# The way back of an attention mix: identity and gate weights in one matmul, or a transpose and a matmul of 16 columns

## The chip, the cores and the metric

One Trainium2 chip, one core of it. The metric is the time of one launch in device microseconds (us). The kernel before took 448.68 us, the median of three runs (448.59 to 450.16).

## What is computed

Attention over a window of 128 keys, then a mixture of experts on its rows. Cut to what matters:

```python
# q, k, v: [4, 8, 576, 64]
scores = scale * q @ k.T + bias            # masked outside a window of 128
attn = softmax(scores)
x = (attn @ v).transpose(0, 2, 1, 3).reshape(2304, 512)
logits = x @ w_gate                        # [2304, 8]
expert = argmax(logits); gate = softmax(logits)[expert]
out[i] = gate[i] * (relu(x[i] @ w1[expert]) @ w2[expert])
```

Everything is float32. The choice of expert hangs on `logits`, so neither `x` nor the gate product may lose precision.

## The kernel before, in words

The kernel has two stages. In the attention stage (some 12 to 172 us of the profile) each of the 4 batches is cut into 5 units of queries, four of 128 rows and one of 64, and each unit into two quads of 4 heads: `STEPS` = 10 steps in a batch, 40 in all, numbered `kk` in a batch. The expert stage follows; its matmuls all stand on L1286, and the change touches nothing in it.

Every engine's order is written out by hand in a loop over the steps. In step `kk` TensorE (PE) does, in this order (`batch`, L1197):

1. `turn_q` or `turn_k` (L1104): four transposes of rows of a unit that is due two units later, into bank 7 of PSUM. It waits for `back_kept`, since bank 7 also holds the result of the way back.
2. `turn_probs` (L1139): eight transposes (four for the first unit) of the probabilities of this step.
3. `turn_back` (L1169) of the step before, the place of the change. It waits for `mixT_ready`, and ahead of it PE waits for the copy of what it turned in 1: `kT_ready` (VectorE, L769) in the odd steps, `qT_ready` (ScalarE, L609) in the even ones.
4. `score` (L1126) of two steps later: four matmuls.
5. `mix` (L1158): eight matmuls (four for the first unit) that give the mix of heads transposed, `mixT`, features on the partitions and queries in the columns.

`turn_back` brings the mix back to rows and forms the gate's partial products at once. The right operand `eye_wg` has 144 columns for each chunk of 128 features: the identity in 128 of them, and 16 columns of gate weights (2 heads x 8 experts, the rows of the other head being zero).

```python
back_ps = ps[:, 7, 0:2 * PAIR].rearrange("p (c n) -> p c n", c=2)   # PAIR = P + 2 * E = 144
for c in range(2):
    last = te.matmul(back_ps[0:rows[i], c, :], mixT[:, c, 0:rows[i]], eye_wg[:, 2 * quad + c, :], ...)
```

VectorE (DVE) then multiplies both parts with the inverse sums of the softmax (`normalise`, L789 and L795), which is also what frees bank 7 (`back_kept`). In each step DVE does: the copy of turned keys (L769, odd steps), its half of the copies of probabilities (L325), in odd steps `sums_eps` and `inv_sums` (L775, L777), `normalise`, and the four passes that add the bias and take the minimum (L757). ScalarE (ACT) copies `mixT` (L616), turned queries (L609), the other half of the probabilities (L621), and does the exponentials (L602).

GpSimd (POOL) builds the constants at the start, `eye_wg` among them (L474, L475), and later splits the first expert's weights in two parts, eight times a CAST (L506) and a TENSOR_TENSOR (L507), beside the attention. ACT waits for `eye_ready` before it issues the loads of the gate weights into `eye_wg` (L652); PE waits for these (`wg_landed`) once, in step 1.

How a float32 matmul shows in the profile: each one is two MATMUL rows with a weight load (LDWEIGHTS, engine PEld) each; a transpose is one of each. Call such a pair of load and MATMUL a pass. So `turn_back` is four passes in each step, 160 in all.

Of the kernel before, what the change touches and what calls it, by code (L numbers as in the profile page):

```python
# [24 lines left out]
ALU = mybir.AluOpType  # L25
# [3 lines left out]
P = 128  # L29
# [5 lines left out]
def attention_moe(nc, q, k, v, w_gate, w1, w2, capacity, out):  # L35
    B, H, S, DH = q.shape
    D, E = w_gate.shape
# [6 lines left out]
    DC, FC = D // P, F // P  # L44
# [4 lines left out]
    PAIR = P + 2 * E  # L49
# [10 lines left out]
    rows = [min(P, S - P * i) for i in range(TI)]  # L60
# [9 lines left out]
    with ctx:  # L70
        def sb(name, shape, dt=F32):
            return ctx.enter_context(nc.sbuf_tensor(name, shape, dt))
# [9 lines left out]
        def sem(name):  # L82
            return ctx.enter_context(nc.semaphore(name))
# [25 lines left out]
        inv_sums = sb("inv_sums", [P, TI, H])  # L109
        eye_wg = sb("eye_wg", [P, DC, PAIR])  # L110
        gate_part = sb("gate_part", [P, H, E])
# [136 lines left out]
        early_kept = sem("early_kept")  # L248
        eye_ready = sem("eye_ready")
        x_ready = sem("x_ready")  # L250
# [201 lines left out]
        def _(pool):  # L452
            steps = [0]

            def link(ins):

                steps[0] += 1
                ins.then_inc(pool_step, 1)
                pool.wait_ge(pool_step, steps[0])
# [13 lines left out]

            link(g.memset(eye_wg[:, :, :], 0.0))  # L474
            g.affine_select(out=eye_wg[:, :, 0:P], in_=eye_wg[:, :, 0:P], compare_op=ALU.not_equal, fill=1.0,  # L475
                            base=0, pattern=[[0, DC], [-1, P]], channel_multiplier=1).then_inc(eye_ready, 1)

# [115 lines left out]
        def _(act):  # L593
# [55 lines left out]
            nc.scalar.activation(mins[:, 0, 0:1], ident[:, 0:1], ACT.Exp)  # L649
            act.wait_ge(eye_ready, 1)  # L650
            for part in range(2):
                act.dma_start(eye_wg[DH * part:DH * part + DH, :, P + E * part:P + E * part + E],  # L652
                              w_gate.rearrange("(c t p) e -> t p c e", t=2, p=DH)[part]).then_inc(wg_landed, 16)
# [437 lines left out]
        def _(pe):  # L1091
# [72 lines left out]
            def turn_back(b, kk):  # L1164

                i, quad = divmod(kk, 2)
                pe.wait_ge(mixT_ready, b * STEPS + kk + 1)
                for c in range(2):
                    last = te.matmul(back_ps[0:rows[i], c, :], mixT[:, c, 0:rows[i]], eye_wg[:, 2 * quad + c, :],  # L1169
                                     start=True, stop=True)  # L1170
                last.then_inc(turned_back, 1)
# [237 lines left out]
```

## Time and profile before

| | |
|---|---|
| median of 3 runs | 448.68 us |
| profiled execution, its own time | 449.06 us |
| span of the profile | 447.4 us |
| PE busy | 422.8 us, 95% |
| DVE, ACT, POOL busy | 279.3, 217.6, 98.6 us |
| share of PE in the chain that ended last | 86% |
| all passes of L1169 | 29.0 us busy, 160 of them |

The span leaves out what lies around the program's instructions: the profiled execution took 1.7 us more than its span. Matmuls are pipelined, so that the durations of neighbours overlap: what a pass costs in a stream is the distance from one start to the next, not its duration.

### The profile page before, as it was taken

How to read it: one execution, taken by the hardware profiler on the slowest of the kernel's cores; microseconds unless marked ns; L12 is line 12 of the kernel's file. 1: busy time of each engine (PE TensorE's matmuls, PEld its weight loads, DVE VectorE, ACT ScalarE, POOL GpSimd, SP SyncE). 2: the span in 40 equal slices, each digit the busy share in tenths (PEclk: the TensorE clock that was granted, in tenths of full speed). 3: DMA queues.
4: the chain of work that ended last, by engine and by line, in shares of the span. 5: the costliest groups of instructions: out<-in, count | busy, mean ns of one | idle time of the engine just before them, and what ended most of it. 6: DMA issues, size and time to landing. Idle time of an engine off the chain costs nothing.

```text
span 447.4 us, 11059 instructions
## 1 busy us (share of the span) xinstructions
PE 422.8 (95%) x2860; PEld 342.1 (76%) x2861; DVE 279.3 (62%) x829; ACT 217.6 (49%) x576; POOL 98.6 (22%) x154
## 2 busy tenths in 40 slices
PE   6999999999999989799999999999999999999982
PEld 6777687777777767688888888888888888888871
DVE  4887778778879776676776634662667766432230
ACT  3777677676677671434455515422444555111100
POOL 5092065000501201222122222222111122222201
PEclk9999999999999999999999999999999999999997
DMA  9997299269631111166566651660656664111100
GB/s 175 242 257 190 70 270 225 73 195 228 147 74 46 49 26 37 48 235 219 177 206 213 201 180 50 225 234 26 216 188 193 216 206 134 47 47 37 36 35 15
DMA packets 78861, 63.59 MB, mean 142 GB/s; under 512 B 61614, under 2 KB 61614, under 8 KB 78832
## 3 DMA queue, kind: packets, MB, share of 16 engines
q1 hardware_dynamic: 71504, 51.66, 41.1%
q0 software_dynamic: 3520, 10.76, 7.5%
q10 hardware_dynamic: 3808, 0.80, 1.1%
q8 instruction: 15, 0.25, 0.2%
q14 instruction: 14, 0.11, 0.1%
HBM read 53.77 MB, written 10.23 MB: 143 GB/s over the span
## 4 chain that ended last, share of the span: by engine, by line
PE 86%; DVE 7%; DMA 2%; ACT 1%; issue 1%; SPq 0%; POOL 0%; DVEq 0%; POOLq 0%
PE ps L1286 52%; PE ps L1126 7%; PE ps L1158 7%; PE ps L1169 5%; PE ps L1139 4%; PE ps L1303 4%; PE ps L1104 3%; DVE probs L757 2%; PE ps L1279 2%; DMA q_rows<-in_q 2%; DVE kT L769 1%; ACT qT L609 1%; DVE sums_eps L775 1%; PE ps L1193 1%; DVE probsT L325 0%
## 5 line engine op out<-in xcount | busy, mean ns | idle before, releaser
L1286 PE MATMUL ps<-weights_sb,rowsT_hi 128*128 (+1 forms) x336 | 107.8, 402 | 1.4 <-DVE rowsT_lo L1024 1.4
L1286 PE MATMUL ps<-weights_sb,hiddenT_hi 128*128 x320 | 98.6, 389 | 1.2 <-DVE hiddenT_lo L1017 1.2
L695 ACT ACTIVATE hidden<-ps 128x512 f32<-128x512 f32 x20 | 11.9, 597 | 139.7 <-PE ps L1286 100.7
L1037 DVE TENSOR_TENSOR weights_sb<-raw,weights_sb 128x1024 f32 (+1 forms) x56 | 67.2, 1221 | 15.7 <-issue 10.9
L602 ACT ACTIVATE probs<-probs,mins 128x256 f32<-128x256 f32 (+2 forms) x160 | 73.7, 467 | 0.0
L1286 PEld LDWEIGHTS ps<-weights_sb,rowsT_hi 128*128 128x128 f32 x336 | 61.1, 188 | 15.2 <-DVE rowsT_lo L1024 1.6
L1286 PEld LDWEIGHTS ps<-weights_sb,hiddenT_hi 128*128 128x128 f32 x320 | 60.0, 188 | 14.0 <-issue 1.4
L1286 PE MATMUL ps<-weights_sb,rowsT_lo 128*128 (+1 forms) x168 | 66.2, 394 | 0.0
L1286 PE MATMUL ps<-weights_sb,hiddenT_lo 128*128 x160 | 62.4, 390 | 0.0
L1017 DVE TENSOR_TENSOR hiddenT_lo<-ps,hiddenT_hi 128x512 fp32r<-128x512 f32 x40 | 25.8, 686 | 58.0 <-ACT hiddenT_hi L699 58.0
L684 ACT ACTIVATE weights_sb<-raw 128x1024 f32 (+1 forms) x56 | 56.6, 1067 | 0.0
L757 DVE CUSTOM_DVE_ANT_0 probs<-ps,bias 128x256 f32<-128x256 f32 (+2 forms) x160 | 51.7, 378 | 6.2 <-PE ps L1126 5.8
L552 POOL DMA_INDIRECT out<-y_sb,dst_now x20 | 20.3, 1015 | 154.3 <-DVE y_sb L1044 154.3
L1126 PE MATMUL ps<-kT,qT 64*128 64x256 f32 (+2 forms) x320 | 39.9, 368 | 1.0 <-DVE kT L769 1.0
L1158 PE MATMUL ps<-probsT,v_rows 128*64 128x128 f32 (+2 forms) x576 | 40.5, 272 | 0.1
L1158 PEld LDWEIGHTS ps<-probsT,v_rows 128*64 128x64 f32 (+1 forms) x576 | 30.1, 135 | 13.1 <-issue 9.6
L1286 PEld LDWEIGHTS ps<-weights_sb,rowsT_lo 128*128 128x128 f32 x168 | 31.5, 187 | 7.7
L1169 PE MATMUL ps<-eye_wg,mixT 128*128 128x144 f32 (+1 forms) x160 | 29.0, 304 | 7.8 <-DVE kT L769 4.8
L1139 PE MATMUL ps<-ident,probs 128*128 128x128 f32 (+2 forms) x288 | 35.7, 264 | 0.0
L1286 PEld LDWEIGHTS ps<-weights_sb,hiddenT_lo 128*128 128x128 f32 x160 | 30.0, 188 | 6.3
L1044 DVE TENSOR_SCALAR y_sb<-ps,weight_now 128x512 f32<-128x512 f32 x20 | 15.0, 751 | 30.2 <-PE ps L1286 29.9
L325 DVE COPY probsT<-ps 128x512 f32<-128x512 f32 (+3 forms) x48 | 23.8, 509 | 15.4 <-PE ps L1139 15.3
(152 smaller groups left out, 532.5 us busy)
## 6 DMA issues: line engine op xcount, KB each, us to landing
raw<-in_moe_w SPq DMA_DIRECT2D x64, 512.0 KB, 3.8
q_rows<-in_q SPq DMA_DIRECT2D x16, 256.0 KB, 5.7
v_rows<-in_v SPq DMA_DIRECT2D x16, 256.0 KB, 4.3
x_rows<-x_sb SPq DMA_DIRECT2D x16, 256.0 KB, 4.1
k_rows<-in_k SPq DMA_DIRECT2D x13, 256.0 KB, 5.7
k_rows<-in_k ACTq DMA_DIRECT2D x3, 256.0 KB, 5.8
q_rows<-in_q SPq DMA_DIRECT2D x4, 128.0 KB, 4.1
k_rows<-in_k SPq DMA_DIRECT2D x4, 128.0 KB, 4.4
```

The lines of the kernel that those rows point to most:

```text
L325: last = copy(dst[0:size, lo:hi, :, 0:rows[i]], src[0:size, lo:hi, :, 0:rows[i]])
L552: g.indirect_dma_start(out, bass.IndirectOffsetOnAxis(ap=dst_now[j][:, 0:1], axis=0), y_sb[j][:, :], None, bounds_check=N - 1, oob_is_err= ...
L602: last = nc.scalar.activation(pr, pr, ACT.Exp, bias=mins[0:rows[i], kk % 2, n:n + 1], scale=-1.0, accum_out=sums[0:rows[i], i, h:h + 1])
L684: nc.scalar.activation(weights_sb[:, bass.ds(e & 1, 1), 2 * layer, RAW * j:RAW * (j + 1)] .rearrange("p s n -> p (s n)"), raw[:, j, :], AC ...
L757: last = vec.tensor_tensor_reduce(out=probs[0:rows[i], kk % 2, n, 0:keys[i]], in0=src, in1=bias[0:rows[i], head(quad, n), shift:shift + ke ...
L1017: vec.tensor_tensor(hiddenT[1][:, 4 * half:4 * half + 4, :], hiddenT_ps(half).rearrange("p (c s) -> p c s", c=4), upper, ALU.subtract).the ...
L1037: vec.tensor_tensor(weights_sb[:, slot, 2 * layer + 1, part].rearrange("p s n -> p (s n)"), raw[:, j, :], weights_sb[:, slot, 2 * layer, p ...
L1126: ins = te.matmul(scores_ps(kk % 2, odd)[0:rows[i], 256 * n:256 * n + keys[i]], qT[part, i, h // 2, 0:rows[i]], kT[part, h // 2, first_key ...
L1139: last = te.transpose(probsT_ps(odd)[0:size, at:at + rows[i]], probs[0:rows[i], kk % 2, 2 * odd + n, P * blk:P * blk + size], ident[0:rows ...
L1158: last = te.matmul(mixT_ps[DH * odd:DH * odd + DH, n, 0:rows[i]], v_rows[0:size, tile, DH * h:DH * h + DH], probsT[0:size, blk, 2 * odd + ...
L1169: last = te.matmul(back_ps[0:rows[i], c, :], mixT[:, c, 0:rows[i]], eye_wg[:, 2 * quad + c, :], start=True, stop=True)
L1286: ins = te.matmul(dst, left[a], right[c], start=first and n == 0, stop=last and n == 2)
```

## The change

`turn_back` now first turns the two chunks of `mixT` back with two transposes against `ident`, the identity that the other transposes use, and then multiplies each chunk with the 16 columns of gate weights alone, in matmuls of their own, into the columns behind. The results lie where they lay. The table `eye_wg` is replaced by `wg_pairs`, which has the 16 columns for each of four chunks; POOL only clears it, and the building of four identities is gone. The rest of the diff renames the semaphore.

```diff
-        eye_wg = sb("eye_wg", [P, DC, PAIR])
+        wg_pairs = sb("wg_pairs", [P, DC, 2 * E])
...
-            link(g.memset(eye_wg[:, :, :], 0.0))
-            g.affine_select(out=eye_wg[:, :, 0:P], in_=eye_wg[:, :, 0:P], compare_op=ALU.not_equal, fill=1.0,
-                            base=0, pattern=[[0, DC], [-1, P]], channel_multiplier=1).then_inc(eye_ready, 1)
+            g.memset(wg_pairs[:, :, :], 0.0).then_inc(wg_cleared, 1)
...
-            act.wait_ge(eye_ready, 1)
+            act.wait_ge(wg_cleared, 1)
             for part in range(2):
-                act.dma_start(eye_wg[DH * part:DH * part + DH, :, P + E * part:P + E * part + E],
+                act.dma_start(wg_pairs[DH * part:DH * part + DH, :, E * part:E * part + E],
                               w_gate.rearrange("(c t p) e -> t p c e", t=2, p=DH)[part]).then_inc(wg_landed, 16)
...
                 pe.wait_ge(mixT_ready, b * STEPS + kk + 1)
+                back = back_ps
                 for c in range(2):
-                    last = te.matmul(back_ps[0:rows[i], c, :], mixT[:, c, 0:rows[i]], eye_wg[:, 2 * quad + c, :],
+                    te.transpose(back[0:rows[i], c, 0:P], mixT[:, c, 0:rows[i]], ident[:, :])
+                for c in range(2):
+                    last = te.matmul(back[0:rows[i], c, P:PAIR], mixT[:, c, 0:rows[i]], wg_pairs[:, 2 * quad + c, :],
                                      start=True, stop=True)
                 last.then_inc(turned_back, 1)
```

On PE the order of a step in the second unit of a batch reads, before:

```order
L1104 MATMUL ps<-ident,k_rows 128x64 x4
L1139 MATMUL ps<-ident,probs 128x128 x8
L1169 MATMUL ps<-eye_wg,mixT 128x144 x2
L1126 MATMUL ps<-kT,qT 128x256 x4
L1158 MATMUL ps<-probsT,v_rows 64x128 x8
```

and now:

```order
L1102 MATMUL ps<-ident,k_rows 128x64 x4
L1137 MATMUL ps<-ident,probs 128x128 x8
L1168 MATMUL ps<-ident,mixT 128x128 x2
L1170 MATMUL ps<-wg_pairs,mixT 128x16 x2
L1124 MATMUL ps<-kT,qT 128x256 x4
L1156 MATMUL ps<-probsT,v_rows 64x128 x8
```

Two rows stand where one stood; nothing changed its place, and the same holds in all 40 steps. In passes, four became six: two of a transpose, four of a matmul.

On POOL the start reads, before:

```order
L471 AFFINE_SELECT maskadd<-maskadd 128x256
L474 MEMSET eye_wg 128x576
L475 AFFINE_SELECT eye_wg<-eye_wg 128x4x128
L479 IOTA iota_e 128x8
```

and now:

```order
L471 AFFINE_SELECT maskadd<-maskadd 128x256
L474 MEMSET wg_pairs 128x64
L477 IOTA iota_e 128x8
```

One instruction is gone and one is smaller; ACT's loads of the gate weights wait for the last of these.

## Rows read from the trace of the kernel before

**Rows 1.** The page: busy time of the engines, and PE's clock in 40 slices.

```profile
PE 422.8 (95%) x2860; PEld 342.1 (76%) x2861; DVE 279.3 (62%) x829; ACT 217.6 (49%) x576; POOL 98.6 (22%) x154
...
PEclk9999999999999999999999999999999999999997
```

**Rows 2.** The chain that ended last, 12 to 172 us, its shares by line.

```profile
by line: PE ps L1126 20.6%; PE ps L1158 18.3%; PE ps L1169 15.3%; PE ps L1139 12.1%; PE ps L1104 9.3%; DVE probs L757 6.6%; DVE kT L769 3.8%; issue 2.4%; ACT qT L609 2.3%; DVE sums_eps L775 1.9%; DVE probsT L325 1.3%; DVE x_sb L789 0.8%; PE
```

**Rows 3.** Timeline of PE, two steps: start us, us, engine, line, what, count.

```profile
62.73 0.76 PE L1169 MATMUL ps<-eye_wg,mixT 128*128 128x144 f32 x4
63.42 1.13 PE L1126 MATMUL ps<-kT,qT 64*128 64x256 f32 x8
...
66.83 0.66 PE L1169 MATMUL ps<-eye_wg,mixT 128*128 128x144 f32 x4
67.42 1.13 PE L1126 MATMUL ps<-kT,qT 64*128 64x256 f32 x8
```

**Rows 4.** The chain in order of time, pieces of PE: start us, us, what.

```profile
148.45 0.22 PE ps L1139 x2
148.67 0.49 PE ps L1169 x4
...
149.19 0.34 PE ps L1177 x14
```

**Rows 5.** Timeline of weight loads: the first two of four blocks (L1169, L1104, L1169).

```profile
22.77 0.30 PEld L1169 LDWEIGHTS ps<-eye_wg,mixT 128*128 128x128 f32 x2
...
21.33 0.20 PEld L1104 LDWEIGHTS ps<-ident,k_rows 128*128 128x128 f32 x2 [0.17 <-issue]
...
47.23 0.19 PEld L1169 LDWEIGHTS ps<-eye_wg,mixT 128*64 128x64 f32 x2 [0.33 <-DVE kT L769]
```

**Rows 6.** A group of weight loads by shape: busy us, mean ns | idle before.

```profile
L1169 PEld LDWEIGHTS ps<-eye_wg,mixT 128*128 128x128 f32 x128 | 17.4, 189 | 10.3 <-DVE kT L769 6.0 <-DVE rowsT_lo L880 1.6 <-issue 0.8
```

**Rows 7.** Timeline of weight loads: four transposes of 64 rows of queries.

```profile
65.51 0.33 PEld L1104 LDWEIGHTS ps<-ident,q_rows 64*128 64x128 f32 x4 [0.17 <-issue]
```

**Rows 8.** Timeline of PE: a way back of the unit of 64 rows.

```profile
50.91 0.70 PE L1169 MATMUL ps<-eye_wg,mixT 128*64 128x144 f32 x4 [0.25 <-ACT qT L609]
51.54 0.70 PE L1126 MATMUL ps<-kT,qT 64*128 64x256 f32 x4
```

**Rows 9.** Timeline of DVE, POOL and PE about 31 to 34 us.

```profile
31.01 2.37 POOL L507 TENSOR_TENSOR weights_sb<-raw,weights_sb 128x1024 fp32r<-128x1024 f32 x1
...
31.67 1.73 DVE L775 TENSOR_SCALAR sums_eps<-sums 128x8 f32<-128x8 f32 x1
...
34.26 0.33 PE L1104 MATMUL ps<-ident,q_rows 128*128 128x128 f32 x1 [0.65 <-DVE gate_part L795]
```

**Rows 10.** The same about 71 to 74 us, and POOL and DVE about 63 us.

```profile
71.63 1.46 DVE L775 TENSOR_SCALAR sums_eps<-sums 128x8 f32<-128x8 f32 x1
...
73.94 0.33 PE L1104 MATMUL ps<-ident,q_rows 128*128 128x128 f32 x1 [0.38 <-DVE gate_part L795]
...
62.71 1.04 POOL L506 CAST weights_sb<-raw 128x1024 fp32r<-128x1024 f32 x1
63.83 2.37 POOL L507 TENSOR_TENSOR weights_sb<-raw,weights_sb 128x1024 fp32r<-128x1024 f32 x1
...
63.47 0.31 DVE L775 TENSOR_SCALAR sums_eps<-sums 128x8 f32<-128x8 f32 x1
```

**Rows 11.** Timeline of ACT at the start.

```profile
4.44 0.20 ACT L649 ACTIVATE mins<-ident 128x1 f32<-128x1 f32 x1
4.57 1.37 ACTq L652 DMA_DIRECT2D eye_wg<-in_moe_w_gate  x2
```

**Rows 12.** Timeline of PE at the start.

```profile
1.63 3.54 PE L1258 MATMUL ps<-ident 128*128 128x128 f32 x16 [1.63 <-POOL ident L463]
5.54 0.66 PE L1104 MATMUL ps<-ident,q_rows 128*128 128x128 f32 x4 [0.37 <-DMA q_rows<-in_q]
6.03 0.60 PE L1104 MATMUL ps<-ident,k_rows 128*128 128x128 f32 x4
```

More of the change, by code:

```diff
@@ L248, in attention_moe @@
         early_kept = sem("early_kept")
-        eye_ready = sem("eye_ready")
+        wg_cleared = sem("wg_cleared")
         x_ready = sem("x_ready")
```

## The prediction

> **What bounds the kernel now.** I read the page first, then the chain of waits for the attention stage, then the timeline of single steps, and last the groups of weight loads. On the page the reader is to see that TensorE (PE) is busy for 95% of the span and that its granted clock stays at the upper of its two levels, 2.4 GHz, up to the last slice [rows 1]. The chain shows the same for the stage that the change touches: of the 160 us from 12 to 172, PE's five lines hold 75.6%, and the way back alone, L1169, 15.3% [rows 2]. Of its 40 blocks I count 37 in the chain. So what a block gets longer or shorter, the stage mostly does too. It is not enough to compare durations, since passes overlap. The prices below are distances between starts.
>
> **What one block costs now.** A block that follows on without a wait takes 0.49 us for four passes, 0.122 each, while a transpose takes 0.11 [rows 4]. From its first start to that of the next block, at L1126, are 0.59 us, as from 66.83 to 67.42 [rows 3]; so 0.10 goes to handing over to `score`, whose operands have another shape. A block that begins after a wait takes 0.69, as from 62.73 to 63.42 [rows 3]: its first weight load isn't hidden. How long a load occupies the array can be read there. The second load starts when the first matmul starts, when the first load is done. Two loads of 0.19 span 0.30, so the second began 0.11 after the first; for a transpose the same reading gives 0.20 less 0.14, 0.06; for the unit of 64 rows 0.19 less 0.136, 0.054 [rows 5]. This is what the diff doesn't show: **the load of a float32 matmul takes 0.108 for 128 columns of weights, twice that of a transpose, and it takes this whatever the matmul moves**. Now it hides behind the 144 columns moved: the loads last 189 ns by their mean, and yet a pass takes 0.122 [rows 4, 6].
>
> **What a block costs after the change.** Two transposes, 0.22. Then four passes with 16 columns, each still with a load of its own. Moving 16 columns takes 16/144 of 0.122, 0.014, too short to hide a load of 0.108: the pass is as long as its load. How much above the load a pass lies that its load bounds is seen in transposes that move 64 columns: (0.33 - 0.14)/3 = 0.063 for a load of 0.057 [rows 5, 7]. So I take 0.108 + 0.006 = 0.114. After a wait: first load 0.057, transpose 0.109, transpose with the first gate load behind it 0.114, three more passes 0.342, the last stream 0.014, handing over 0.09: 0.73 for 0.69, **+0.04**. Without a wait the first load is hidden in both, and it is 0.67 for 0.59, **+0.09**. In the unit of 64 rows (two steps of ten) it is 0.63 now [rows 8]; loads are half as long, a gate pass takes about 0.062, and the sum is 0.03 + 0.109 + 0.109 + 0.186 + 0.014 + 0.09 = 0.54, **-0.10**.
>
> No row shows a float32 pass of 16 columns, so both ends are kept. Below: a pass of 0.063, as if the gate loads were as quick as those of transposes [rows 7]; further off, 0.024, as in the bf16 matmuls of 8 to 48 columns [rows 4]. Above: 0.122, as now, whatever is moved or loaded [rows 4]. I take 0.114, since the 0.108 under it is measured on the very operand that is loaded, `mixT`.
>
> **The sum.** Of the 37 blocks in the chain, 24 are of full rows and begin after a wait, 5 without one (pieces of 0.49 like that in rows 4), 8 are of 64 rows. Not all of it arrives. About 31.7 us DVE's `sums_eps` lies for 1.73 us instead of 0.16 and ends when POOL's TENSOR_TENSOR ends; PE then waits 0.65 for bank 7 [rows 9]. POOL's work there starts when the raw weights land, not when PE is ready. What the four blocks ahead add (3 x 0.04 + 0.09 = 0.21) only makes this stall shorter. The same stands at 71.6 us, with 0.38 of waiting [rows 10]. POOL's second group is set off by a load that waits for the end of the first batch, so only the three blocks since then count, 0.17, and they vanish too. Left are 19 x 0.04 + 3 x 0.09 - 8 x 0.10 = 0.76 + 0.27 - 0.80 = **+0.2 us**. The three blocks off the chain stand beside DVE work (the two stalls, and the choice of the expert's top at 98 us) and cost nothing; without that cover they would add 0.2.
>
> The other edits. POOL's second constant falls away and ACT may issue the gate loads sooner, but ACT is busy with its first ACTIVATE until 4.64 and issues from 4.57 [rows 11]: nothing to gain, and the cover is that instruction. DVE reads the result as before, 0.04 to 0.09 later, in a step where it sits idle for longer than that. 40 x 2 more passes have to be issued; a pass of 0.024 [rows 4] shows that issuing isn't a limit. No queue of transfers and no other wait moves.
>
> Against the profiled execution of 449.06 the sum gives 449.3; that execution lies 0.4 above the median shown. Against the median it is 448.68 + 0.22 = **448.9 us**.
>
> **The rivals.**
> *A, gate passes as cheap as they look.* What speaks for it: 16 columns for 144. If a gate pass costs 0.063, a full block is 0.12 (0.08) shorter than now: 19 x 0.12 + 3 x 0.08 + 0.8 = 3.4 us gained, 445.3; with 0.024 some 443. Against it stand the loads of 0.108 [rows 5]. The Trainium skill, page "Perfetto Trace Analysis", section "Transposes", asks that a logical transpose be a transpose and not a standard matmul; by it the change is an improvement, and 445.3 is its time. It leaves out that the operand must now be loaded twice. I give A 8%.
> *B, a fixed price for each pass.* If a pass costs 0.122 whatever it loads, a block after a wait gets 0.07 longer, one without 0.12, and the unit of 64 rows gains nothing and gets 0.09 longer: 19 x 0.07 + 3 x 0.12 + 8 x 0.09 = 2.4, **451.1 us**. It decides from the point where a pass of 16 columns and 64 columns of weights costs more than 0.12. For it: every pass of L1169 takes 0.122 now, with 64 columns of weights too. Against it: 144 columns moved explain that, and the transposes show 0.063 [rows 7]. I give B 12%.
> *C, the clock falls.* After the change PE moves 0.43 us less by matmul in a step and more by transpose. If transposes don't keep the clock up, PE falls from 2.4 to 1.2 GHz. A transpose at the lower level takes 3.54/16 = 0.22, as the sixteen of the start show [rows 12]; twice the PE share of rows 2 would be 120 us more, 569. But those sixteen are all that PE had done, and right behind them four transposes take 0.49 with their first load, 0.11 each: transposes alone raised the clock [rows 12]. The Trainium skill, page "TensorE: Matmul & The Clock Gate", section "Part 4: PE-mode transpose", says that the upper level isn't reached by transposes, which don't count as busy; by that rule the time is that of C, and the trace disagrees. 2%.
> *D, another meeting with POOL.* At 63.47 `sums_eps` waits 0.15 for the end of a CAST; the next TENSOR_TENSOR starts at 63.83 [rows 10]. If DVE came 0.3 later it would lie behind all 2.37 of it. I expect 0.04 later. The stall of 1.57 at 31.7 cost PE 0.65, so this one would cost about 1.4, 450.3: within the bound of no difference. It is part of the forecast's 78% and widens its range.
>
> **How the numbers follow.** The forecast's own terms give 448.4 (a pass of 0.109: 19 x 0.02 + 3 x 0.06 - 0.8 = -0.3) to 449.6 (0.122 for full rows only: +0.9), and D adds up to 1.4; the three runs shown reach from 448.6 to 450.2, so chance alone can move the time by half a microsecond. I take 447.5 to 451.0 for 8 in 10; it leaves out A, C and most of B. What differs by 0.5%, 2.2 us, can be told from no change: faster than 446.4 is A, 8%; slower than 450.9 is B and C, 14%; the rest, 78%, is no difference.
>
> **What would show it.** The gate passes' loads should have a mean of about 189 ns (136 for 64 rows) and begin 0.11 apart, the whole block with the two transposes taking 0.67 or 0.73, and 0.54 in the unit of 64 rows. Passes 0.06 apart are A, 0.122 in the unit of 64 rows too is B. PE's clock should stay up. The stall near 31.7 should be 0.2 shorter and end at the same time. The shares of DVE and ACT should not move. I would be wrong most if the load of a narrow matmul is not the 0.108 that I read off a first load, or if the blocks of 64 rows gain nothing.

## The result, and the profile after

The changed kernel takes 452.89 us, the median of 18 runs (449.54 to 455.13); the kernel before took 449.1 us beside it (18 runs, 448.04 to 450.16). The ratio is 1.0073, with a 95% interval of 1.0051 to 1.0095. The quotient of the medians is 1.0084, that of the means 1.0074. So it is slower by 0.73%, more than the bound of no difference (0.5%), and the time lies above the predicted range.

| | before | after |
|---|---|---|
| median | 449.1 us | 452.89 us |
| profiled execution, its own time | 449.06 us | 455.13 us |
| span of the profile | 447.4 us | 453.4 us |
| PE busy | 422.8 us | 429.3 us |
| mean granted clock of PE in it | 0.994 | 0.985 |

The page of the kernel after:

```profile
span 453.4 us, 11217 instructions
...
PE 429.3 (95%) x2940; PEld 350.9 (77%) x2941; DVE 279.5 (62%) x829; ACT 217.6 (48%) x576; POOL 99.4 (22%) x153
...
PEclk9999999999999986999999999999999999999998
```

The shares of the engines stand where they stood [rows 1], and so do the shares of the chain from 12 to 172 us; the way back, now two lines, has 15.5% of it (15.3% in [rows 2]):

```profile
by line: PE ps L1124 20.6%; PE ps L1156 18.1%; PE ps L1137 12.7%; PE ps L1102 9.3%; PE ps L1168 7.8%; PE ps L1170 7.7%; DVE probs L755 6.6%; DVE kT L767 3.8%; issue 2.3%; ACT qT L607 2.3%; DVE sums_eps L773 1.9%; DVE probsT L325 1.4%; DVE x
```

What is new is an 8 and a 6 in the line of the clock, in slices 15 and 16 of 40, some 160 to 180 us: there TensorE ran at the lower of its two levels for part of the time. The kernel before shows nothing like it.

So there are two effects, and the timeline of the two profiled executions keeps them apart. I compare the start of the same way back in both:

| step (of 40, from 0) | before | after | difference |
|---|---|---|---|
| 34 | 154.03 | 155.54 | +1.5 |
| 35 | 159.72 | 161.26 | +1.5 |
| 36 | 163.16 | 166.24 | +3.1 |
| 38 | 168.67 | 171.94 | +3.3 |
| first matmul behind the stage | 174.20 | 180.34 | +6.1 |
| end of the span | 447.4 | 453.4 | +6.0 |

At the first way back of all, ahead of any new block, the difference is 0.16 (15.06 for 14.90). So up to 160 us the longer blocks have made at most 1.35. Then come two jumps, of 1.5 and of 2.9, and behind the stage the difference stays the same. Both jumps are stretches at the lower level. Windows of the kernel after (stretch, length; busy us and count of PE, PEld, DVE, ACT, POOL; then granted clock, transfers' share and GB/s):

```profile
157.00:163.00 6.00, 4.62 (x50) 3.54 (x48) 3.85 (x16) 3.42 (x11) 1.21 (x2) 1.00 0.00 0
163.10:166.40 3.30, 3.30 (x24) 2.97 (x20) 1.21 (x9) 1.15 (x3) 0.00 (x0) 0.50 0.32 80
166.50:173.20 6.70, 6.70 (x83) 5.28 (x81) 5.38 (x25) 4.62 (x22) 0.00 (x0) 1.00 0.12 43
173.40:180.00 6.60, 6.60 (x25) 4.82 (x24) 2.13 (x11) 0.28 (x1) 0.00 (x0) 0.50 0.09 20
```

and of the kernel before, at the same places of the program:

```profile
155.50:161.50 6.00, 4.62 (x50) 3.46 (x48) 3.93 (x16) 3.42 (x11) 1.19 (x2) 1.00 0.01 3
161.50:164.90 3.40, 3.40 (x42) 2.76 (x40) 2.70 (x15) 2.36 (x9) 0.00 (x0) 1.00 0.30 78
164.90:171.40 6.50, 6.47 (x74) 4.73 (x70) 4.33 (x23) 3.79 (x17) 0.00 (x0) 1.00 0.11 42
```

The eighth number is to be read. It is 0.50, 1.2 GHz, for 3.4 us from 163.0, and for 6.8 us from 173.3. Beside the first numbers it is instructive: ahead of the first fall PE was busy for 4.62 of 6.00 us in both kernels, and ahead of the second one for 6.70 of 6.70. **By the busy share nothing was amiss; the clock fell all the same, and only after the change.** What a fall costs is read in the timeline around the first. After:

```profile
161.26 0.44 PE L1168 MATMUL ps<-ident,mixT 128*128 128x128 f32 x2 [1.38 <-DVE rowsT_lo L878]
161.53 0.52 PE L1170 MATMUL ps<-wg_pairs,mixT 128*128 128x16 f32 x4
...
162.78 1.77 PE L1156 MATMUL ps<-probsT,v_rows 128*64 128x128 f32 x16
164.48 1.97 PE L1137 MATMUL ps<-ident,probs 128*128 128x128 f32 x8
166.24 0.49 PE L1168 MATMUL ps<-ident,mixT 128*128 128x128 f32 x2
```

The same place before:

```profile
161.20 1.09 PE L1158 MATMUL ps<-probsT,v_rows 128*64 128x128 f32 x16
162.23 1.09 PE L1139 MATMUL ps<-ident,probs 128*128 128x128 f32 x8
163.16 0.66 PE L1169 MATMUL ps<-eye_wg,mixT 128*128 128x144 f32 x4
```

From start to start the mix takes 1.70 us and the eight transposes 1.76, for 1.03 and 0.93 before. That is 1.5 more, all of the first jump.

The block itself, in the kernel after, first of full rows, then of 64 rows:

```profile
23.00 0.44 PE L1168 MATMUL ps<-ident,mixT 128*128 128x128 f32 x2
23.27 0.52 PE L1170 MATMUL ps<-wg_pairs,mixT 128*128 128x16 f32 x4
23.72 0.49 PE L1124 MATMUL ps<-kT,qT 64*128 64x256 f32 x2
...
51.45 0.41 PE L1168 MATMUL ps<-ident,mixT 128*64 128x128 f32 x2 [0.25 <-ACT qT L607]
51.78 0.40 PE L1170 MATMUL ps<-wg_pairs,mixT 128*64 128x16 f32 x4
52.12 0.49 PE L1124 MATMUL ps<-kT,qT 64*128 64x256 f32 x2
```

From start to start the first takes 0.72, 0.69 before [rows 3], and the second 0.67, 0.63 before [rows 8]. The block of 64 rows got longer, where I had forecast 0.10 less. Its weight loads say why:

```profile
22.99 0.20 PEld L1168 LDWEIGHTS ps<-ident,mixT 128*128 128x128 f32 x2
23.16 0.53 PEld L1170 LDWEIGHTS ps<-wg_pairs,mixT 128*128 128x128 f32 x4
...
51.44 0.14 PEld L1168 LDWEIGHTS ps<-ident,mixT 128*64 128x64 f32 x2 [0.49 <-ACT qT L607]
51.78 0.31 PEld L1170 LDWEIGHTS ps<-wg_pairs,mixT 128*64 128x64 f32 x4 [0.20 <-issue]
```

With full rows the first gate load begins at 23.16, while the second transpose is still moving. With 64 rows the transposes' loads end at 51.58 and the next begins only at 51.78, with 0.20 us in which nothing is loaded. By an estimate from 0.11 for a transpose, the second one begins to move at 51.56 and is through at 51.67, 0.11 ahead of that load.

The passes themselves cost what was forecast. Their loads, in groups by shape (busy us, mean ns | idle before), stand beside the 189 of [rows 6]:

```profile
L1170 PEld LDWEIGHTS ps<-wg_pairs,mixT 128*128 128x128 f32 x128 | 16.8, 192 | 0.0
...
L1170 PEld LDWEIGHTS ps<-wg_pairs,mixT 128*64 128x64 f32 x32 | 2.7, 146 | 1.8 <-issue 1.8
```

How far apart they begin is read from the block above: four of them (0.53) less the last one's 0.19 make three distances of 0.113; with 64 rows (0.31 - 0.146)/3 makes 0.055. The 1.8 us of idle time in the second group, over the 8 blocks of 64 rows, are the gap: 0.2 each.

Of the 18 runs 8 had a mean granted clock of 0.993 or more; they took 449.54 to 451.75, a median of 450.1, 1.0 above the kernel before (two of them, at 451.7, stand apart, and no trace of them was kept). Five had 0.987 or 0.988 and took 452.86 to 454.13. Five had 0.984 or 0.985 and took 454.29 to 455.13. **The longer passes cost about 1.0 us, and the 10 runs of 18 with a lower clock took 2.8 to 5.0 more (3.0 and 4.6 by the medians of the two groups).** The median, 452.89, is that of a time with three values; the experiments had to say where both costs come from.

### The profile page after: what moved, and what is told of

Read it like the earlier page. It is cut to its first block, busy times and chain, and to the rows that moved or that the text cites. A ratio compares the mean times of both kernels' runs of the same rounds, so it can differ in the third digit from the quotient of the medians.

```text
span 453.4 us, 11217 instructions
## 1 busy us (share of the span) xinstructions
PE 429.3 (95%) x2940; PEld 350.9 (77%) x2941; DVE 279.5 (62%) x829; ACT 217.6 (48%) x576; POOL 99.4 (22%) x153
## 2 busy tenths in 40 slices
DMA packets 78862, 63.61 MB, mean 140 GB/s; under 512 B 61614, under 2 KB 61614, under 8 KB 78832
## 4 chain that ended last, share of the span: by engine, by line
PE 87%; DVE 7%; DMA 2%; ACT 1%; issue 1%; SPq 0%; POOL 0%; DVEq 0%; POOLq 0%
PE ps L1287 52%; PE ps L1124 7%; PE ps L1156 7%; PE ps L1137 5%; PE ps L1304 4%; PE ps L1102 3%; PE ps L1168 3%; PE ps L1170 3%; DVE probs L755 2%; PE ps L1280 2%; DMA q_rows<-in_q 2%; DVE kT L767 1%; ACT qT L607 1%; DVE sums_eps L773 1%; PE ps L1194 1%
## 5 line engine op out<-in xcount | busy, mean ns | idle before, releaser
L1287 PE MATMUL ps<-weights_sb,rowsT_hi 128*128 (+1 forms) x336 | 109.6, 408 | 1.4 <-DVE rowsT_lo L1022 1.4
L1035 DVE TENSOR_TENSOR weights_sb<-raw,weights_sb 128x1024 f32 (+1 forms) x56 | 67.2, 1220 | 15.5 <-issue 8.8
L1287 PEld LDWEIGHTS ps<-weights_sb,rowsT_hi 128*128 128x128 f32 x336 | 62.1, 191 | 15.3 <-DVE rowsT_lo L1022 1.6
L1156 PE MATMUL ps<-probsT,v_rows 128*64 128x128 f32 (+2 forms) x576 | 41.5, 276 | 0.1
L1137 PE MATMUL ps<-ident,probs 128*128 128x128 f32 (+2 forms) x288 | 36.7, 268 | 0.0
L1137 PEld LDWEIGHTS ps<-ident,probs 128*128 128x128 f32 (+2 forms) x288 | 30.0, 139 | 2.2 <-issue 1.5
```

The source lines that it names most:

```text
L1035: vec.tensor_tensor(weights_sb[:, slot, 2 * layer + 1, part].rearrange("p s n -> p (s n)"), raw[:, j, :], weights_sb[:, slot, 2 * layer, p ...
L1137: last = te.transpose(probsT_ps(odd)[0:size, at:at + rows[i]], probs[0:rows[i], kk % 2, 2 * odd + n, P * blk:P * blk + size], ident[0:rows ...
L1156: last = te.matmul(mixT_ps[DH * odd:DH * odd + DH, n, 0:rows[i]], v_rows[0:size, tile, DH * h:DH * h + DH], probsT[0:size, blk, 2 * odd + ...
L1287: ins = te.matmul(dst, left[a], right[c], start=first and n == 0, stop=last and n == 2)
```

## The experiments

The theory behind the first four: the gate passes cost what their loads cost (1.0 us), and the clock falls where too little is moved through the array, near 163 and 173 us. Its rivals: the clock falls by chance wherever the kernel has become longer, or because of the longer stage ahead of it.

In tables "fell" counts the runs with a mean granted clock under 0.992. A fall of 3.4 us to the lower level takes 3.4 x 0.5 / 450 = 0.004 from the mean, and runs without one lie at 0.993 to 0.996, so a run of 0.992 or 0.993 can hide one short fall; only the profiled runs show it for certain. Each kernel's runs stand beside runs of the kernel before on the same chip.

**e1: the new form in the last batch alone.** Batches 0 to 2 have the old form. In this one and in the others with both forms the table stays `eye_wg`, and the gate weights are its last 16 columns.

```diff
+                if b == B - 1:
+                    for c in range(2):
+                        te.transpose(back_ps[0:rows[i], c, 0:P], mixT[:, c, 0:rows[i]], ident[:, :])
+                    for c in range(2):
+                        last = te.matmul(back_ps[0:rows[i], c, P:PAIR], mixT[:, c, 0:rows[i]],
+                                         eye_wg[:, 2 * quad + c, P:PAIR], start=True, stop=True)
+                else:
+                    for c in range(2):
+                        last = te.matmul(back_ps[0:rows[i], c, :], mixT[:, c, 0:rows[i]],
+                                         eye_wg[:, 2 * quad + c, :], start=True, stop=True)
```

> The old way back in batches 0 to 2, the new one in the last batch alone. The trace of the changed kernel has the granted clock at its lower level for 3.4 us from 163.0 and for 6.8 us from 173.3, both at the end of the last batch, which the trace of before has not. Theory 1 (the new way back keeps PE less occupied with moving, and at the end of the last batch, where PE waits for VectorE and there are no more scores, that lets the clock fall): runs scatter as those of the changed kernel do, from about 449 to 454 us, and a share of them has a mean granted clock of 0.988 or 0.985 instead of 0.994. Rival 2 (the falls need the whole of the changed kernel, since all of it runs later or is moved against the chip's own rhythm): hardly any falls, 449.0 to 449.7 us. Rival 3 (a disturbance of those runs that has nothing to do with the kernel): the runs of before beside these fall as often.

**e2: the new form in batches 0 to 2, the old one in the last.** The same edit with `b < B - 1`.

> The complement: the new way back in batches 0 to 2, the old one in the last batch. Theory 1: no falls, mean clock 0.994 in every run, and only the longer blocks stay: three quarters of the 1.4 us by which the changed kernel is behind at 154 us, so before plus 1.0 to 1.2, about 450.2 us, with a scatter like that of before. Rival 2: falls in a share of the runs, up to 454 us.

| | median (range) | runs | ratio | fell |
|---|---|---|---|---|
| e1, new in the last batch | 451.59 (449.52 to 452.71) | 6 | 1.0037 (1.0017 to 1.0058) | 4 |
| e2, old in the last batch | 450.25 (449.91 to 450.85) | 4 | 1.0015 (1.0003 to 1.0028) | 0 |

A quarter of the new blocks brings the falls (451.54 to 452.71 in the four runs that fell, 449.52 and 449.85 in the two that did not), and three quarters of them elsewhere bring none. The profile of e1, by windows:

```profile
160.00:169.80 9.80, 9.80 (x119) 7.85 (x119) 7.62 (x39) 6.07 (x26) 0.00 (x0) 1.00 0.19 55
170.00:176.60 6.60, 6.60 (x24) 4.75 (x22) 2.04 (x11) 0.28 (x1) 0.00 (x0) 0.50 0.10 22
```

PE was busy for all of 9.80 us ahead of this fall. So the new form in the last batch alone is enough for a fall, and longer blocks ahead of it aren't needed. That falls stand nowhere else is not shown: e2 has only four runs, and the profiles of e4, e9 and e10 below each have a fall in batch 2, from 114.1, 130.7 and 112.3. e2 shows the price of the passes alone: +0.6 for three quarters of the blocks.

Its profile says little about the stalls. `sums_eps` starts at 31.84 and lies for 1.47 instead of 1.73, and PE then waits 0.30 for bank 7 instead of 0.65. But e1, whose first three batches are the old ones, has 1.51 and 0.42 there: the stall moves by 0.2 from one execution to the next without any change. At 71.6 PE waits in neither. Instead `sums_eps` of e2 lies for 1.71 at 63.61, and PE waits 0.41: that is rival D.

**e3: the old form for the units of 64 rows.** `if rows[i] == P:` the new form, else the old one.

> The new way back for units of 128 rows, the old one for the units of 64 rows, in all batches. In the changed kernel a block of 64 rows takes 0.675 us against 0.634 before, where I had forecast 0.54: 8 blocks, so this should give back about 0.3 us. If the blocks of 64 rows are also what lets the clock fall the second time (two of them stand right before 173.3), the runs with a fall should get rarer or have only the shorter one, and the median should come down to 450 to 451 us. If it is the full ones as well, the median stays at 452 to 453.

**e4: the gate matmuls of all units in the full array.** In the units of 64 rows, 128 columns of `mixT` are loaded as weights, and 128 rows written.

```diff
-                    last = te.matmul(back[0:rows[i], c, P:PAIR], mixT[:, c, 0:rows[i]], wg_pairs[:, 2 * quad + c, :],
+                    last = te.matmul(back[:, c, P:PAIR], mixT[:, c, :], wg_pairs[:, 2 * quad + c, :],
```

> The changed kernel, but in the units of 64 rows the gate matmuls load all 128 columns of the mix and write all 128 rows (the lower 64 are never read). In the changed kernel's trace there is a gap of 0.09 us between the last transpose and the first gate load in these blocks, and none in the full ones. Theory (the gap is a change of the array's shape: a float32 matmul with 64 columns of weights is run in half the array, the transposes in all of it): the gap is gone, the gate passes are 0.111 apart instead of 0.058, and the block takes about 0.66 to 0.70 us. Rival (the transpose of 64 columns itself ends late): the gap stays, and the block takes about 0.79 us.

e3 took 450.87 (6 runs, 449.84 to 452.55), ratio 1.0035 (1.0018 to 1.0051); two fell. Two of 6 can't be told from 10 of 18, so that the share of the blocks of 64 rows in the falls stays open. Its blocks of 64 rows are back at 0.63. Its profiled execution, in which the clock did not fall, shows the meeting with POOL that I had called rival D. POOL, DVE and PE about 64 to 67 us:

```profile
63.92 2.36 POOL L507 TENSOR_TENSOR weights_sb<-raw,weights_sb 128x1024 fp32r<-128x1024 f32 x1
63.96 2.35 DVE L775 TENSOR_SCALAR sums_eps<-sums 128x8 f32<-128x8 f32 x1
...
67.16 0.46 PE L1104 MATMUL ps<-ident,q_rows 64*128 64x64 f32 x4 [1.05 <-DVE gate_part L795]
```

DVE's `sums_eps` began 0.04 us behind POOL's instruction and lay for all of it; PE waited 1.05.

e4 was run once: 454.87 us, with the clock down for 3.4 us from 114.1 and for 6.8 from 172.2. It met POOL as e3 did, `sums_eps` lying for 2.00 at 63.60 and PE waiting 0.70. Its block of 64 rows is what it was made for:

```profile
50.92 0.41 PE L1168 MATMUL ps<-ident,mixT 128*64 128x128 f32 x2 [0.25 <-ACT qT L607]
51.16 0.52 PE L1170 MATMUL ps<-wg_pairs,mixT 128*128 128x16 f32 x4
51.61 0.49 PE L1124 MATMUL ps<-kT,qT 64*128 64x256 f32 x2
```

The gap between the last transpose and the first gate load is gone: the gate passes begin 0.24 after the transposes, not 0.33. With twice the columns to load, the four passes then take 0.45 up to `score`, not 0.34, and so the block is 0.69 in all. The 0.09 belongs to the step from a transpose to a float32 matmul with 64 columns of weights, not to the transposes of 64 rows, which are the same in e4. The Trainium skill, page "TensorEngine Tiling (Array Packing)", section "Key Properties", says that changing the tiling mode drains TensorE, and its section "Restrictions" that column tiling rules out the transpose mode for FP32 input. The two together would put a gap just here, and the trace has one, of 0.09 us. No row names a mode of the array, so that the gap is shown and its reading as a drain is not.

**What lets the clock fall: three candidates.** 1a: transposes don't keep the clock up, and the new form replaced matmuls by transposes. 1b: what is moved through the array keeps it up, by transposes too, but loading weights does not; the gate passes load for 0.11 and, by the prediction's estimate, move for 0.014. 1c: being busy keeps it up, whatever PE does. Beside these stands the plain rival that only the length of the stage counts. e5 and e6 fill the four steps ahead of and between the falls with passes that move much, and e7 adds passes that only load.

**e5: sixteen transposes more**, four in each of the steps 5 to 8 of the last batch, into a part of bank 7 that nobody reads.

```diff
                 pe.wait_ge(mixT_ready, b * STEPS + kk + 1)
                 back = back_ps
+                if b == B - 1 and 5 <= kk <= 8:
+                    for _ in range(4):
+                        te.transpose(ps[:, 7, 3 * P:4 * P], ident[:, :], ident[:, :])
```

> The changed kernel, and in the last batch's ways back of steps 5 to 8 four transposes of the identity more each, into columns that nobody reads, after the waits and so on PE's path: 16 passes of 0.109, +1.7 us for any theory. Theory 1a (transposes do not keep the clock up): falls as often as in the changed kernel (10 of 18 runs) or more, median 454 to 456. Theory 1b (what a pass moves keeps it up, a transpose too, and the gate passes fail because they mostly load): falls get rare, most runs at 451.5 to 452.5 with a mean clock of 0.993 to 0.996.

**e6: eight matmuls of 128 columns more** in the same places, the same time by other passes.

```diff
+                    for _ in range(2):
+                        te.matmul(ps[:, 7, 3 * P:4 * P], ident[:, :], ident[:, :], start=True, stop=True)
```

> The same as the run with filling transposes, with two float32 matmuls of 128 columns (four passes, 0.109 each) in the place of each four transposes: the same time added, the same columns moved. Theories 1a and 1b both expect hardly any falls, 451.5 to 452.5 us; if falls stay as frequent here, neither holds and the clock doesn't hang on what PE moves at the end of the batch.

**e7: the gate matmuls twice** in all steps of the last batch.

```diff
-                for c in range(2):
+                for c in (0, 1, 0, 1) if b == B - 1 else (0, 1):
                     last = te.matmul(back[0:rows[i], c, P:PAIR], mixT[:, c, 0:rows[i]], wg_pairs[:, 2 * quad + c, :],
```

> The changed kernel, and in the last batch each gate matmul is done twice: 10 blocks of 4 passes more at 0.111 (0.058 for 64 rows), +4.0 us. PE is busier by the clock on the wall, but what is added is loading. Theory 1c (being busy keeps the clock up, whatever PE does): falls get rare, 454 to 455 us. Theories 1a and 1b (loading doesn't count): every run or nearly every run falls, and more of the stretch is slow: 458 us or more, mean clock 0.985 or lower.

| | median (range) | runs | ratio | fell |
|---|---|---|---|---|
| after | 452.89 (449.54 to 455.13) | 18 | 1.0073 (1.0051 to 1.0095) | 10 |
| e5, transposes added | 452.81 (451.73 to 453.48) | 6 | 1.0072 (1.0053 to 1.0092) | 0 |
| e6, matmuls added | 453.05 (451.91 to 453.86) | 6 | 1.0081 (1.0060 to 1.0101) | 0, one at 0.992 |
| e7, gate matmuls doubled | 458.08 (456.52 to 460.70) | 6 | 1.0199 (1.0168 to 1.0230) | 6 |

The two windows of 10 us about the second fall tell the same. Of e5:

```profile
163.00:173.00 10.00, 10.00 (x118) 8.48 (x117) 6.75 (x34) 6.20 (x26) 0.00 (x0) 1.00 0.17 50
173.20:183.30 10.10, 10.08 (x92) 7.34 (x90) 6.38 (x35) 1.00 (x3) 1.47 (x2) 1.00 0.09 15
```

and of e7:

```profile
163.00:173.00 10.00, 10.00 (x118) 8.54 (x116) 6.52 (x32) 6.20 (x27) 0.00 (x0) 1.00 0.13 34
173.20:183.30 10.10, 10.10 (x53) 7.19 (x53) 3.40 (x17) 0.45 (x3) 0.00 (x0) 0.50 0.10 27
```

The first lines can hardly be told apart: the same busy time, and the same number of matmuls and loads within one. In a full step the added passes take the same 0.44 us in both. What differs is what they move, 128 columns in the added passes of e5 and 16 in those of e7. Behind the one the clock stays, behind the other it falls, for 10.1 us, and so it went in all runs, 0 of 6 against 6 of 6. This is 1b. 1a is refuted by e5: by it the falls should have stayed as frequent as after the change. The matmuls of e6 did as well, but for one run of 0.992, which may hide a short fall. 1c is refuted by e7, where PE was as busy. The length of the stage isn't it either: it is longer in e5 than after the change, and no run of e5 fell.

e5 is longer than a run of the kernel after that kept its clock by more than its added passes. Those take 0.44 in each of four steps, 1.75; the profiled execution was already 1.1 us behind after's at 147 us, ahead of all of them. Of that, 0.57 was there at its first way back, at 15.63 us. It then met POOL, and PE waited 1.01 for bank 7 at 27 us, as e6's did with 0.67; that is the meeting of [rows 9] at another step, and later waits differ too. Neither is made by the added passes.

**e8: the kernel before without `sums_eps`.** Was the meeting with POOL worth something in the kernel before? The reciprocal is taken of the sums directly.

```diff
-                vec.tensor_scalar(sums_eps[0:r, i, :], sums[0:r, i, :], 1e-9, None, ALU.add).then_inc(sum_step, 1)
-                dve.wait_ge(sum_step, b * 2 * TI + 2 * i + 1)
-                vec.reciprocal(inv_sums[0:r, i, :], sums_eps[0:r, i, :]).then_inc(sum_step, 1)
+                vec.reciprocal(inv_sums[0:r, i, :], sums[0:r, i, :]).then_inc(sum_step, 1)
```

> The kernel before without the addition of 1e-9 to the sums of exponentials (a sum is at least 1, so that the addition changes no bit); the reciprocal reads the sums themselves. In the traces the addition lay behind POOL's weight splitting for 0.5 to 2.3 us, and cost PE up to 1.1 us in one place and 0.4 to 0.65 in others. Theory (it is this instruction that is held while POOL works): the stalls of 0.65 and 0.38 us in the trace of before are gone, and the short wait between the two operations too: 1.0 to 1.5 us less than before, 448.2 to 448.7, and less scatter. Rival (the reciprocal is held in its place): no change.

It took 448.12 us (12 runs, 447.62 to 448.79), ratio 0.9973 (0.9963 to 0.9984), and in six more runs later the same 448.12, ratio 0.9972 (0.9960 to 0.9984):

> The kernel without the addition of 1e-9 once more, on the same chip as the run with the new order, so that the two can be compared: 0.25 to 0.3% below before, 12 runs within 1.2 us of one another.

POOL and DVE in the profile of e8, at the place of [rows 9]:

```profile
31.17 2.37 POOL L507 TENSOR_TENSOR weights_sb<-raw,weights_sb 128x1024 fp32r<-128x1024 f32 x1
...
31.45 0.19 DVE L775 RECIPROCAL inv_sums<-sums 128x8 f32<-128x8 f32 x1
```

The reciprocal begins inside POOL's instruction and takes 0.19. It is not held, where the TENSOR_SCALAR was held for 1.73. Where the time was won is seen by setting the ways back of the two profiled executions beside each other. e8 is 0.22 ahead at the first one, ahead of any stall; 0.94 behind the wait of 0.65 at 34 us, 1.40 behind that of 0.38 at 74 us [rows 9, 10], and 1.41 at the end of the stage. So it is the two waits, 0.7 and 0.45; the small instruction that each unit does without on DVE wins nothing elsewhere.

**e9: the order transpose, gate, transpose, gate.** If a gate load can hide behind a transpose that moves, each of the two should have one.

```diff
                 for c in range(2):
                     te.transpose(back[0:rows[i], c, 0:P], mixT[:, c, 0:rows[i]], ident[:, :])
-                for c in range(2):
                     last = te.matmul(back[0:rows[i], c, P:PAIR], mixT[:, c, 0:rows[i]], wg_pairs[:, 2 * quad + c, :],
```

> The changed kernel with the four operations of the way back in another order: transpose of the first chunk, its gate matmul, transpose of the second, its gate matmul, instead of both transposes and then both matmuls. Theory (a gate pass is as long as its weight load of 0.108 unless a transpose's moving of 0.107 lies over that load): two loads are hidden now instead of one, at the price of one short load of a transpose that isn't: a block of 128 rows after a wait takes 0.67 instead of 0.72 us (0.688 with the old way back), one without a wait 0.61 instead of 0.665 (0.586). A block of 64 rows changes the array's shape three times instead of once and takes about 0.85 instead of 0.675. Rival (the order doesn't matter, every pass has its price): 0.72, 0.665 and 0.675 as in the changed kernel.

```profile
22.68 0.33 PE L1168 MATMUL ps<-ident,mixT 128*128 128x128 f32 x1
22.85 0.29 PE L1169 MATMUL ps<-wg_pairs,mixT 128*128 128x16 f32 x2
22.99 0.30 PE L1168 MATMUL ps<-ident,mixT 128*128 128x128 f32 x1
23.13 0.29 PE L1169 MATMUL ps<-wg_pairs,mixT 128*128 128x16 f32 x2
23.35 0.49 PE L1124 MATMUL ps<-kT,qT 64*128 64x256 f32 x2
...
47.43 0.30 PE L1168 MATMUL ps<-ident,mixT 128*64 128x128 f32 x1 [0.17 <-DVE kT L767]
47.66 0.29 PE L1169 MATMUL ps<-wg_pairs,mixT 128*64 128x16 f32 x2
47.88 0.30 PE L1168 MATMUL ps<-ident,mixT 128*64 128x128 f32 x1
48.11 0.29 PE L1169 MATMUL ps<-wg_pairs,mixT 128*64 128x16 f32 x2
48.33 0.38 PE L1124 MATMUL ps<-kT,qT 64*128 64x128 f32 x2
```

This is PE's timeline of e9, a single run of 458.68 us with a mean clock of 0.972 (down for 10.2 us from 130.7 and again from 175.1). A full block takes 0.67, 0.02 less than before the change [rows 3] and 0.05 less than after it. The block of 64 rows goes three times from a transpose to a narrow matmul or back and takes 0.90. The full block loads as much in less time, and in this run the clock fell for longer, which cost more than the order won; one run doesn't show that the order made it so.

**e10: e8 and this order for the full units of batches 0 to 2; e12: for batches 0 and 1 only.** The last batch, and all units of 64 rows, keep the old form.

```diff
                 for c in range(2):
+                    if b < B - 1 and rows[i] == P:
+                        te.transpose(back_ps[:, c, 0:P], mixT[:, c, :], ident[:, :])
+                        last = te.matmul(back_ps[:, c, P:PAIR], mixT[:, c, :], eye_wg[:, 2 * quad + c, P:PAIR],
+                                         start=True, stop=True)
+                    else:
+                        last = te.matmul(back_ps[0:rows[i], c, :], mixT[:, c, 0:rows[i]],
+                                         eye_wg[:, 2 * quad + c, :], start=True, stop=True)
```

> The kernel before without the addition of 1e-9, and with the way back as transpose, gate matmul, transpose, gate matmul, but only for units of 128 rows of batches 0 to 2; units of 64 rows and the whole last batch, where the clock is at stake, keep the one matmul of 144 columns. If a block after a wait takes 0.67 for 0.688 and one without 0.61 for 0.586: 18 x 0.02 - 3 x 0.03 = 0.25 us less than without the addition alone, 0.3% and a little below before; no falls of the clock. If the loads aren't hidden by the order: 0.7 us more than without the addition alone.

> The last kernel (no addition of 1e-9; transpose, gate matmul, transpose, gate matmul) with the new way back in batches 0 and 1 alone. One of its five runs had the clock down for 3.4 us from 112.3, right behind the step of batch 2 in which PE waits 1.1 us for VectorE's routing work, and took 449.75 us instead of 447.5 to 448.0. If the clock falls where a wait and the new way back come together, no run falls now, since in batches 0 and 1 there is no such wait: all runs within 447.5 to 448.3 us. If the falls come by chance with the new way back anywhere, one or two of the runs are at 449.5 or more.

| | median (range) | runs | ratio | fell |
|---|---|---|---|---|
| e8, no `sums_eps` | 448.12 (447.62 to 448.79) | 12 | 0.9973 (0.9963 to 0.9984) | 0 |
| e10, and in turn in batches 0 to 2 | 447.80 (447.49 to 449.75) | 5 | 0.9961 (0.9947 to 0.9975) | 1 |
| e12, and in turn in batches 0 and 1 | 448.18 (447.39 to 448.52) | 10 | 0.9961 (0.9949 to 0.9973) | 0 |

The intervals of all three overlap. That they are faster than both kernels of this case is shown; that the order in turn adds something to e8 is not. One run of e10 fell, the profiled one, in batch 2:

```profile
105.50:112.30 6.80, 5.67 (x67) 4.77 (x65) 5.46 (x25) 5.25 (x19) 1.15 (x2) 1.00 1.17 226
112.30:115.60 3.30, 3.30 (x21) 2.48 (x22) 1.72 (x9) 0.34 (x2) 3.30 (x7) 0.50 0.69 169
```

There PE had just waited 1.13 us for a copy of DVE. The fall of e4 in batch 2 begins right behind the same wait (1.13 us, up to 113.39), and the first one of after 1.7 us behind a wait of 1.38. The second fall of after and those of e1 and e7 have none ahead of them. Whether the wait or the blocks let the clock fall in batch 2 isn't shown: e12 does without the place and fell in none of 10 runs, but with one fall in five, as in e10, ten runs without one come by chance one time in ten.

## Why the prediction was wrong

**What held.** The reading that nothing in the diff shows, that a float32 load of 128 columns occupies the array for 0.108 and that a gate pass therefore costs 0.114 whatever it moves, held: 0.113 measured after the change and 0.111 in e7, whose eight gate passes take 0.89 up to the next block, and 0.055 for 64 columns where I had 0.062. A full block got longer by 0.03 after a wait (forecast +0.04) and by 0.08 to 0.09 without one (forecast +0.09). Rival A (passes of 0.063) and rival B (0.122 for 64 columns too) both fell by these numbers. Issuing 80 more passes cost nothing to be seen, and the other edits nothing either: the page shows DVE and ACT as they were.

**What failed first: the term of the units of 64 rows.** It was -0.10 for each of 8 blocks, in a sum of +0.2. Measured is +0.04. In the row of its parts, "0.03 + 0.109 + 0.109 + 0.186 + 0.014 + 0.09", one is missing: from a transpose to a float32 matmul with 64 columns of weights 0.09 us pass. e4 shows it by loading 128 columns instead, without the gap. I had counted a hand-over of 0.09 at the end of the block, to `score`, whose operands have another shape, and not asked whether the block now has one inside. With the measured prices the sum of the 30 blocks that I had let arrive is 19 x 0.033 + 3 x 0.08 + 8 x 0.041 = 1.2 us, and the runs that kept their clock are 1.0 above the kernel before. This alone would have given 450.1, inside the range and no difference by the bound.

**What failed most: rival C, at 2%.** "PE's clock should stay up" was wrong in 10 of 18 runs. I argued that transposes alone had raised the clock at the start [rows 12]. I had read that off their price, 0.22 and then 0.11, since the granted clock is listed as 1.00 all through those sixteen; the price agrees with the 0.22 of the eight transposes in the fall at 164.48. e5 bears the argument out: transposes do count. But it answers whether transposes count, and the question was what the four gate passes do, which load for 0.11 and move for 0.014. I had these two numbers in the same text, and had even written that PE moves 0.43 us less by matmul in a step. A sum by time moved would have been: before, four passes of 0.12 each; after, two of 0.11 and four of 0.014, so some 0.21 us less per step. The Trainium skill, page "TensorE: Matmul & The Clock Gate", section "Part 4: PE-mode transpose", says that transposes don't count as busy and don't bring the upper level. By it e5 should have fallen as after the change did; 0 of 6 runs did. It forecast the right sign for a reason that the runs contradict.

The price of C was as wrong as its chance: I priced it for the whole stage, 569 us, a time so far off that the rival was easy to dismiss. A fall is local. It lasted 3.4 to 10.2 us in these runs, and cost 1.5 and 2.9 in the profile of after. With that price, C is a case of 452 to 455 us, and with a chance well above 2% the range would have reached there.

**What held in part.** The stall near 31.7 should have been 0.2 shorter. In the profile of after PE still waited 0.63, not 0.65 - 0.21 = 0.44, because in that execution POOL's instruction began 0.40 later as well:

```profile
31.41 2.36 POOL L505 TENSOR_TENSOR weights_sb<-raw,weights_sb 128x1024 fp32r<-128x1024 f32 x1
32.01 1.80 DVE L773 TENSOR_SCALAR sums_eps<-sums 128x8 f32<-128x8 f32 x1
...
34.65 0.33 PE L1102 MATMUL ps<-ident,q_rows 128*128 128x128 f32 x1 [0.63 <-DVE gate_part L793]
```

POOL's start hangs on when the raw weights land, and that moves from one execution to the next. In e2 the stall cost 0.30, but in e1, where nothing ahead of it is changed, 0.42, and in e5 it stood at another step; no run isolates the 0.2. The stall at 71.6 went from 0.38 to 0.29, not to nothing. All waits of PE behind POOL together made 1.03 in the profile before, 0.92 in that of after, 0.42 in e1 and 1.77 in e3, a scatter of over a microsecond that the term of 0.2 drowns in. Rival D did not come in the profile of after, but in those of e2, e3 and e4, where `sums_eps` lay for 1.71, 2.35 and 2.00 us and PE waited 0.41, 1.05 and 0.70. It was rightly inside the range, and belongs there for either kernel.

**The range.** Its upper end of 451.0 came from the terms of passes and from D. With the clock at its upper level it would have held 6 of the 8 runs, and the median of these. What it left out was a mechanism with two values, which moves a median by 3 us where it strikes in half of the runs.

What stays open: whether the falls of after at 163 and at 173 us come from the same deficit (e7, with more loads still, has only the second), and why some runs of one kernel fall and others don't. Small shifts of DVE and POOL from run to run may be the cause; no experiment isolated it. The kernel before isn't far from the edge either: of the 53 of its runs whose clock is listed, one fell, to 0.989, with 450.7 us.

## What to carry to other kernels

A matmul that is made narrower wins nothing more once its weight load is longer than what it moves; look at the distance of loads, not at columns. Before splitting a wide matmul, count for each part what it moves and what it only loads: an engine that is busy for 100% of the time with loads can lose its clock, and the fall costs more than the passes. Price such a case by local falls of some microseconds, in some of the runs, and give it room in the range.

## What the runs showed of the hardware

- **The clock of TensorE can fall while the profile shows it busy without a gap**: 0.50 behind 10.00 of 10.00 us in e7, behind 9.80 of 9.80 in e1, while 10.00 of 10.00 with more columns moved kept 1.00 in e5. The share of busy time doesn't say which it will be.
- **Transposes keep it up**: with sixteen of them added in e5 no run of 6 fell, where 10 of 18 fell without them; eight float32 matmuls in their place (e6) did about as well, with one doubtful run of 6.
- **Falls lasted about 3.4, 6.8 or 10.2 us** in every profile of this case that has one. The times of the changed kernel lie in groups that go with the mean clock (0.993 and more, 0.987 and 0.988, 0.984 and 0.985).
- **From a transpose to a float32 matmul with 64 columns of weights 0.09 us pass**; with 128 columns of weights there is no such gap.
- **DVE's TENSOR_SCALAR on 128x8 float32 waits for the end of POOL's TENSOR_TENSOR, up to 2.35 us; a RECIPROCAL of the same size takes 0.19 beside it.** The Trainium skill, page "SBUF — State Buffer", section "SBUF: two separate sides", describes a port pair shared by VectorE and GpSimd that an operation of VectorE in a 2-port mode must own alone for its whole length. The trace agrees that the one which starts second waits for the whole of the other: at 31.67 the TENSOR_SCALAR starts 0.66 behind POOL and ends with it, at 33.4. That the TENSOR_SCALAR is in such a mode, and that the reciprocal needs no second port, is my reading of 1.73 and 0.19 us.
